# Three batch loops written out in the code of four engines instead of run as loops

## The reference

```python
# 1: local attention; q, k, v: 4 batches x 8 heads x 768 x 64, chunks of 32 rows
for c in range(24):
    k_full = concat(mem_k, k[c*32-16 : c*32+40]);  v_full likewise
    a = softmax(q_c @ k_full.T / 8);  out_c = a @ v_full
x = out as 3072 x 512
# 2: h = x @ w_in (512 x 1024)
solu = h * softmax(h);  ln = (solu - mean) / sqrt(var + 1e-6) * g_ln
x = ln @ w_out (1024 x 512)
# 3: h = x @ moe2_w_in (512 x 2048)
g = h * clip(h + 3, 0, 6) / 6
result = g @ moe2_w_out (2048 x 512)
```

## Time and profile before

| what | value |
|---|---|
| median of three runs | 946.51 us |
| profiled execution | 949.08 us |
| its span (first to last instruction) | 947.3 us |
| TensorE busy | 902.4 us, 95% |
| VectorE busy | 674.4 us, 71% |
| ScalarE busy | 471.2 us, 50% |
| GpSimd busy | 268.6 us, 28% |
| mean granted TensorE clock | 0.976 |

### The profile page before, as it was taken

The page is one execution under the profiler, slowest core; times in us unless marked ns, Lnnn a source line. Parts: engine busy times, 40 slices in busy tenths (PEclk is TensorE's granted clock), DMA queues, the critical chain, the costliest instruction groups (busy, mean ns, idle before and its releaser), DMA issues.

```text
span 947.3 us, 17198 instructions
## 1 busy us (share of the span) xinstructions
PE 902.4 (95%) x6124; PEld 807.5 (85%) x6124; DVE 674.4 (71%) x1097; ACT 471.2 (50%) x1092; POOL 268.6 (28%) x334
## 2 busy tenths in 40 slices
PE   6879999699997999999999999999999899999998
PEld 5768988589895888889978888888789899999997
DVE  3996878578774677857686555545777978878783
ACT  4675555355554565644675554555653333333320
POOL 3473355435331153462002332323540000000000
PEclk8999999799997999999999999999999999999999
DMA  9643365426743467359573333332987335344441
GB/s 183 143 117 82 79 179 168 153 59 158 221 137 104 100 180 199 122 154 329 190 256 118 127 133 133 129 137 106 341 323 265 117 109 157 97 149 123 140 140 45
DMA packets 146935, 146.84 MB, mean 155 GB/s; under 512 B 96936, under 2 KB 107176, under 8 KB 145832
## 3 DMA queue, kind: packets, MB, share of 16 engines
q1 hardware_dynamic: 133267, 100.29, 36.5%
q0 software_dynamic: 7920, 38.94, 11.7%
q10 hardware_dynamic: 5669, 6.56, 2.1%
HBM read 90.05 MB, written 55.71 MB: 154 GB/s over the span
## 4 chain that ended last, share of the span: by engine, by line
PE 85%; DVE 5%; DMA 5%; issue 3%; ACT 1%; POOL 0%; ACTq 0%; SPq 0%; DVEq 0%; POOLq 0%
PE banks L975 27%; PE banks L1240 23%; PE banks L1023 22%; PE banks L920 3%; PE banks L966 3%; PE banks L928 3%; PE banks L890 2%; PE banks L949 2%; DMA gs_raw<-g_scratch 2%; PE banks L990 1%; DMA ws<-w_split_scratch 1%; DMA xs_raw<-x_scratch 1%; DVE gs_raw L1878 1%; DVE prob L1586 1%; DVE gs L1547 1%
## 5 line engine op out<-in xcount | busy, mean ns | idle before, releaser
L1240 PE MATMUL banks<-vs,gs 128*128 128x256 f32 x2016 | 244.5, 284 | 3.6 <-DVE o_stage L1911 2.9
L1240 PEld LDWEIGHTS banks<-vs,gs 128*128 128x128 f32 x2016 | 243.7, 193 | 4.4 <-DVE o_stage L1911 3.1
L1023 PE MATMUL banks<-xs,ws 128*128 128x512 f32 x1008 | 231.3, 390 | 3.3 <-DMA ws<-w_split_scratch 2.3
L1023 PEld LDWEIGHTS banks<-xs,ws 128*128 128x128 f32 x1008 | 188.2, 188 | 45.0 <-DMA ws<-w_split_scratch 3.2
L1507 ACT CAST gs<-gs_raw 128x1792 fp32r<-128x1792 f32 x48 | 81.4, 1695 | 133.6 <-DVE gs_raw L1878 133.5
L975 PE MATMUL banks<-y_t,w_out 128*128 128x384 f32 x768 | 140.8, 338 | 0.0
L975 PEld LDWEIGHTS banks<-y_t,w_out 128*128 128x128 f32 x768 | 132.2, 188 | 0.7
L975 PE MATMUL banks<-w_in,x_t 128*128 128x512 f32 x504 | 122.5, 399 | 0.0
L975 PEld LDWEIGHTS banks<-w_in,x_t 128*128 128x128 f32 x504 | 94.8, 192 | 20.2
L1298 ACT ACTIVATE prob<-score,small 96x128 f32<-96x128 f32 x256 | 99.3, 392 | 18.7 <-DVE small L1564 17.8
L1878 DVE TENSOR_TENSOR gs_raw<-gs_raw 128x256 f32<-128x256 f32 x192 | 82.6, 431 | 31.6 <-DMA gs_raw<-g_scratch 26.6
(11 more groups left out here) (94 smaller groups left out, 1078.2 us busy)
## 6 DMA issues: line engine op xcount, KB each, us to landing
g_scratch<-part SPq DMA_DIRECT2D x96, 256.0 KB, 2.0
gs_raw<-g_scratch SPq DMA_DIRECT2D x45, 512.0 KB, 3.9
q_in<-in_q_dram SPq DMA_DIRECT2D x32, 192.0 KB, 4.1
x_scratch<-x_out ACTq DMA_DIRECT2D x32, 192.0 KB, 3.5
out_dram<-o_stage SPq DMA_DIRECT2D x12, 512.0 KB, 5.5
k_in<-in_k_dram SPq DMA_DIRECT2D x24, 240.0 KB
v_in<-in_v_dram SPq DMA_DIRECT2D x24, 240.0 KB
v_split_scratch<-v_split POOLq DMA_DIRECT2D x3, 1792.0 KB, 7.8
```

The costliest lines, as they stand in the source:

```text
L1023: mm = pe.matmul(ps, ws[:, W_OF[i], a, kc, :], xs[g][X_OF[i]][:, m, kc, :], start=(fresh and x == 0), stop=(x == len(passes) - 1), skip_gr ...
L1240: mm = pe.matmul(m_ps[i][:, s, :], gs[x][:, a, G_OF[i], s * P:(s + 1) * P], vs[p][:, m, V_OF[i], :], start=(p == 0 and s == 0 and y == 0), ...
```

## The change

In four blocks the loop on the engine becomes a Python loop, so that `batch(1)`, `batch(2)` and `batch(3)` are each put into the engine's list with plain numbers in place of registers. The other three places of the diff are the same as this one:

```diff
@@ -1170,7 +1170,7 @@
             first_batch()
-            with pe.Fori(1, B) as b:
+            for b in range(1, B):
                 batch(b)
             batch(B, last=True)
```

More of the change, by code:

```diff
@@ L453, in _ @@
             first_batch()
-            with sp.Fori(1, B) as b:
+            for b in range(1, B):
                 batch(b)
@@ L1475, in _ @@
             first_batch()
-            with act.Fori(1, B) as b:
+            for b in range(1, B):
                 batch(b)
@@ L1834, in _ @@
             first_batch()
-            with dve.Fori(1, B) as b:
+            for b in range(1, B):
                 batch(b)
```

## The result

The changed kernel takes 922.94 us (median of 4 runs, 921.19 to 924.78) against 946.77 us for the kernel before (4 runs): a ratio of 0.9737, 95% interval 0.9701 to 0.9773. The forecast was 922.6 us. The profiled execution took 923.26 us with a span of 921.4; against 949.08 and 947.3 that is 25.8 us less, 2 us more than between the medians.

The account below looks back on a forecast made before the run. TensorE was taken to set the end, holding 85% of the chain of waits. Savings of 12.68, 10.80 and 0.44 us sum to 23.92; 946.51 − 23.92 gives 922.6 us, range 919.8 to 927.2.

Parts of the forecast that it names:

- a whole step kk = 4 in place of a whole step kk = 0: Batch loop: each step kk = 0 at the jumps and exit should take kk = 4's 10.77 us, winning 23.92 us.
- Jumps of TensorE and ScalarE: Batch loop: removing both engines' taken branches and what follows wins 12.68 us at the first jump, 10.80 at the second.
- SP and VectorE at nothing: Batch loop: these two engines lose jumps that nobody waits for, costed at nothing.
- Straight code at nothing: Written-out batches: added code to fetch costed at 0, since following blocks arrive in time; one late block 3.26 us.
- GpSimd's 12.68 us of slack: After the first jump, GpSimd's idling before line 703 becomes 0, with line 703 starting about when due; cost 0.
- Constants in place of registers: Written-out steps: less register work, taken as 0, with 2.3 us more gain kept as the lower end.
- the exit step: Step kk = 0 where the batch loop is left: 11.21 us, already on constants, forecast to win 0.44 us.
- the branch is only where the time is booked: Rival, batch loop jumps: TensorE really waits for data or VectorE, so no change, 946.5 us; chance 0.03.
- The slower rival: Stage 3's loops, moved in the list, begin to fetch at five jumps, 11.7 us each: 981 us; chance 0.03.
- Part comes back: Rival, shortened steps kk = 0: q or k transfers or GpSimd's weights land too late, 935.6 us; chance 0.06.
- A loop that short stays in the engine, one of 6 blocks doesn't.: TensorE: stage 3's loop of 252 instructions isn't fetched again; the batch loop, 6 to 7 blocks, is fetched every pass.

Follow-up runs that it names:

- the second comparison: The changed kernel timed again against the kernel before, on the same chip as two other kernels: 922.83 us against 947.39, ratio 0.9749.
- the turned loop: Against the kernel before: all batch loops kept, TensorE's body begun one step later, 45 empty instructions ahead of ScalarE's loop; 925.18 us, ratio 0.9764.
- the moved loops: Against the kernel before: all batch loops kept, 120 empty instructions ahead of TensorE's and 45 ahead of ScalarE's; 941.66 us, ratio 0.9918.

## Why the prediction was right

*The size.* 23.92 us forecast, 23.83 between the medians of the first comparison. The way it was reached, a whole step kk = 4 in place of a whole step kk = 0, held to 0.14 us a step. That the totals agree to 0.1 us is luck: the second comparison has 24.56 us, and the runs of the changed kernel alone spread over 3.6 and 7.2 us. Adding up the gaps instead, 3.54 + 3.26 + 2.18 + 3.33 + 3.63 + 0.64 = 16.6 us, would have missed the 7 to 8 us that the low clock takes.

*The parts.* Jumps of TensorE and ScalarE: shown, by one each, by both, and by both kept but moved. SP and VectorE at nothing: shown. Straight code at nothing: shown by the stretches of 91 us, which stayed, and by the turned loop, which fetches 12 blocks fewer and isn't faster. GpSimd's 12.68 us of slack, used up at no cost: seen in the rows above.

*Constants in place of registers.* I took 0 and kept 2.3 us as the lower end. Steps kk = 0 and kk = 4 of the later batches now take 10.63 to 10.68 instead of 10.77, about 0.1 us a step; beyond the 24.3 us counted above that is a few tenths in all. The reason given for 0 was misread: the exit step is shorter too, 11.21 − 0.64 = 10.57 us without its wait.

*The rivals.* That the branch is only where the time is booked fell with the moved loops: the same waits, the same data, and no gap over 0.6 us. On TensorE a branch that falls through takes 0.08 us here, a jump to code that is still there 0.21 to 0.24, and one to code that isn't 3.3 to 3.9; such a jump holds ScalarE for 4 to 9. The Trainium skill (Advanced Engine Details and Errata, section Control Flow Timing) gives about 108 ns for a compare-and-branch; the branch that falls through is near that, the jumps are not. The slower rival, stage 3 beginning to fetch, didn't come: its loops show no instruction packets.

*Part comes back.* As it was written, with a transfer of q or k or GpSimd's weights too late for the short step, it didn't happen: the two rows of waits above name none of them. A wait that grew lies near the start of stage 3. The transfers that prepare it (x_mix_scratch and xs_raw) take their own time, and the chain of the kernel after runs through them:

```profile
401.06 8.38 DMA x_mix_scratch<-x_mix
...
417.36 12.29 DMA xs_raw<-x_scratch
```

TensorE's timeline in that stretch, the one row with a wait for line 1351:

```profile
432.84 2.98 PE L1023 MATMUL banks<-xs,ws 128*128 128x512 f32 x12 [0.91 <-ACT part L1351]
```

The kernel before has no idle time at that place, but waits for line 1351 of 0.17 and 0.37 us a little later. TensorE's waits from the end of the batches to the last stretch, in the kernel before (411.9 to 705):

```profile
PE banks L1023 <- DMA ws<-w_split_scratch: 2.3, 2, 1.8
PE banks L1023 <- ACT part L1351: 1.0, 3, 0.4
```

and in the kernel after (387 to 680):

```profile
PE banks L1023 <- DMA ws<-w_split_scratch: 3.0, 1, 3.0
PE banks L1023 <- ACT part L1351: 1.3, 2, 0.9
```

That is 1.0 us more, most of it in the transfer of ws. In the second profile of the changed kernel the same two waits are 1.7 and 0.7 us, less than before, so no loss is shown here.

*What failed.* One statement in the mechanism was too narrow: "A loop that short stays in the engine, one of 6 blocks doesn't." Not the length alone but the place of the loop decided, and what fits every place tried is the number of blocks touched. By the fetch times, TensorE's loop touched eight blocks of 16 KB and was fetched anew; moved so that it touches seven, it stayed. ScalarE's touched four of 8 KB and was fetched anew; moved to three, it stayed. The block edges are reckoned from when fetches start, and the moves came out as reckoned, but where the edges lie was not read directly. The Trainium skill (Runtime: NRT & Kernel Launch, section Instruction fetch mechanics) speaks of a window of two pages; here seven blocks of TensorE's code and three of ScalarE's stay at hand. The same section of the Trainium skill also gives 128 KiB of instruction memory for TensorE and 32 KiB for most engines; that would be room for eight of TensorE's blocks and four of ScalarE's, in each case one more than the loops that stayed touch.

## What to carry to other kernels

Look at the step after a loop's jump in the trace of every engine: a gap marked "issue" there, with instruction packets in the DMA queues, says that the body is being fetched anew. On TensorE the branch itself took several us; on ScalarE its record stayed short, 45 ns in the kernel before, and only the idle time behind it showed the wait:

```profile
L1476 ACTq COMPARE_BRANCH  x3: 40/45/54, 180.0 to 403.6; - x3
```

Price it by an equal step without a jump, since the clock falls behind the gap and the waits of two engines overlap. Then write the loop out, or move it by turning its body by a step; and don't pad TensorE's list with empty instructions where TensorE is the bound.

## What the runs showed of the hardware that was not expected

An empty instruction on TensorE that only counts up a semaphore is recorded with 0.051 us but they follow each other every 0.15 us.

The step at which the loop is entered, with the same wait of TensorE ahead of it, took 17.04 us in the first profile of the changed kernel and 15.43 in the second, at a granted clock of 0.80 and 0.89. In the first:

```profile
64.92:81.96 17.04, 13.32 (x82) 11.07 (x82) 12.46 (x29) 9.99 (x38) 7.24 (x10) 0.80 0.19 44
```

and in the second:

```profile
64.39:79.82 15.43, 11.72 (x82) 9.57 (x82) 12.32 (x29) 9.90 (x38) 7.27 (x10) 0.89 0.21 48
```

VectorE, ScalarE and GpSimd are busy for the same time in both; TensorE's own work is 1.6 us shorter. Why the clock came back earlier in one than in the other is open; it is part of the spread of the changed kernel's runs (919.42 to 926.65 in the second comparison).
